# Attention followed by two expert layers: fewer filler products beside the mixed tile, expert slots of eight steps, and the first group's rows turned inside the second group's slots

## The reference

```
scores = q @ k.T / sqrt(64)                 # 2 batches, 8 heads, 576 positions, head size 64
kth    = the 32nd largest of each row
attn   = softmax(where(scores >= kth, scores, -1e9))
x      = (attn @ v), heads side by side     # 1152 rows x 512
# first expert layer: one expert of 8 for each row
logits = x @ w_gate + modality_bias[modality_id]
e      = argmax(logits);  g = softmax(logits)[e]
x      = g * (relu(x @ w1[e]) @ w2[e])      # 512 -> 1024 -> 512
# second expert layer: all 4 experts for each row
out    = sum_e p[:, e] * (relu(x @ w1b[e]) @ w2b[e])
```

## Time and profile before

| | us |
|---|---|
| median of two runs | 984.82 |
| the two runs | 984.27 and 985.36 |
| profiled execution, whole | 985.48 |
| its span | 983.7 |
| PE busy | 916.5 (93%) |
| DVE busy | 559.4 (57%) |
| ACT busy | 340.7 (35%) |
| POOL busy | 280.1 (28%) |
| mean granted TensorE clock | 0.946 |

### The profile page before, as it was taken

The page is one execution under the profiler, slowest core; times in us unless marked ns, Lnnn a source line. Parts: engine busy times, 40 slices in busy tenths (PEclk is TensorE's granted clock), DMA queues, the critical chain, the costliest instruction groups (busy, mean ns, idle before and its releaser), DMA issues.

```text
span 983.7 us, 13497 instructions
## 1 busy us (share of the span) xinstructions
PE 916.5 (93%) x4849; PEld 770.0 (78%) x4849; DVE 559.4 (57%) x1100; ACT 340.7 (35%) x726; POOL 280.1 (28%) x224
## 2 busy tenths in 40 slices
PE   4799999987799999995699979999999999999998
PEld 4688888876667767762477868998989898989897
DVE  4999999659998989834655152332314231423121
ACT  3545555433445645531645141221202120212010
POOL 7667665434657665611011030000000000000000
PEclk8579999978989999998699989999999999999999
DMA  9120000000412632533962441020202020000001
GB/s 215 57 94 22 1 23 12 12 11 21 173 34 87 214 108 97 187 114 104 330 216 101 152 179 70 1 83 4 86 1 78 9 85 0 0 0 0 32 11 53
DMA packets 49396, 75.63 MB, mean 77 GB/s; under 512 B 24624, under 2 KB 24624, under 8 KB 49328
## 3 DMA queue, kind: packets, MB, share of 16 engines
q1 hardware_dynamic: 42160, 61.09, 18.2%
q0 software_dynamic: 4160, 13.63, 4.3%
q10 hardware_dynamic: 3008, 0.05, 0.2%
HBM read 63.49 MB, written 11.27 MB: 76 GB/s over the span
## 4 chain that ended last, share of the span: by engine, by line
PE 85%; issue 5%; POOL 4%; DVE 4%; DMA 1%; ACT 1%; ACTq 0%; POOLq 0%; DVEq 0%
PE bank L1270 19%; PE bank L1271 18%; PE bank L1272 18%; PE bank L1326 9%; PE bank L1392 5%; PE bank L1367 4%; PE bank L1265 3%; PE bank L1383 3%; PE bank L1297 3%; POOL att L605 2%; PE bank L1295 2%; POOL att L608 1%; DVE w1l L1152 1%; DMA x_tok<-y_a,a_pos_i 1%; PE bank L1338 1%
## 5 line engine op out<-in xcount | busy, mean ns | idle before, releaser
L605 POOL TENSOR_SCALAR att<-sc,top 128x576 f32<-128x576 f32 x70 | 120.8, 1725 | 149.8 <-DVE top L1011 138.0
L1011 DVE MAX8 top<-work 128x8 f32<-128x576 f32 x216 | 152.4, 745 | 0.1
L1270 PE MATMUL bank<-xT,w1h 128*128 128x384 f32 x384 | 129.5, 337 | 5.3 <-DVE w1l L1152 5.3
L1271 PE MATMUL bank<-xT,w1l 128*128 128x384 f32 x384 | 129.1, 336 | 0.0
L1272 PE MATMUL bank<-xT,w1h 128*128 128x384 f32 x384 | 129.0, 336 | 0.0
L1207 DVE SCALAR_TENSOR_TENSOR hT<-bank,hT 128x384 fp32r<-128x384 f32 x96 | 53.0, 557 | 130.8 <-ACT hT L914 127.3
L914 ACT ACTIVATE hT<-bank 128x384 fp32r<-128x384 f32 x96 | 46.9, 492 | 200.9 <-PE bank L1272 200.9
L1326 PE MATMUL bank<-v_one,attT 128*128 128x65 f32 (+3 forms) x800 | 112.8, 282 | 0.6 <-ACT av L738 0.6
L1270 PE MATMUL bank<-w2h,hT 128*128 128x512 f32 x288 | 112.2, 390 | 1.2 <-DVE hT L1207 1.2
L1326 PEld LDWEIGHTS bank<-v_one,attT 128*128 128x128 f32 (+3 forms) x800 | 98.9, 190 | 17.7 <-issue 10.4
L1272 PE MATMUL bank<-w2l,hT 128*128 128x512 f32 x288 | 112.2, 390 | 0.0
(11 more groups left out here) (239 smaller groups left out, 1520.2 us busy)
## 6 DMA issues: line engine op xcount, KB each, us to landing
w_raw<-in_moe_w_dram SPq DMA_DIRECT2D x96, 512.0 KB, 5.9
q_raw<-in_q_dram SPq DMA_DIRECT2D x18, 128.0 KB, 2.7
v_one<-in_v_dram POOLq DMA_DIRECT2D x18, 128.0 KB, 5.5
out_dram<-x_tok SPq DMA_DIRECT2D x9, 256.0 KB, 2.0
k_raw<-in_k_dram SPq DMA_DIRECT2D x8, 256.0 KB, 5.2
y_dram<-zero POOLq DMA_DIRECT2D x2, 1024.0 KB, 6.6
y_dram<-b_ys POOLq DMA_DIRECT2D x7, 256.0 KB
x_dram<-x_cur SPq DMA_DIRECT2D x6, 256.0 KB, 2.8
```

Source lines behind the costliest of these rows:

```text
L605: nc.gpsimd.tensor_scalar(att[:, g % ATR, :], sc[:, g % RING, :], top8[:, g % RING, 3, 7:8], None, ALU.is_ge).then_inc(keep_made, 1)
L1011: nxt = nc.vector.max(out=top8[:, g % RING, i + 1, :], in_=work[:, j, :])
L1270: nc.tensor.matmul(dst, high_lhs, high_rhs, start=start, stop=False)
L1271: nc.tensor.matmul(dst, low_lhs, high_rhs, start=False, stop=False)
```

## The change

On PE, the number of unread products of a step depends on the tile. On DVE the counter runs with the heads themselves and advances by a seventh after each operation; the chain of group A begins at 34, asks for ranks at 36.6 and for tokens at 39.6. A's slots have eight steps and the fifth begins at step 78. `split_q` runs before the mask of head 8t and `round_q` one step earlier. SP loads the first expert's `w1` after A's fifth slot's up products. POOL gathers B's first two slots ahead of A's rows. The work on A's rows moves into B's slots: the scaling into slots 0 to 2, the turning and splitting into slots 3 to 5. `b_ys` is placed first in its region, over A's `ys`, and DVE's first copy into it waits for A's stores.

```diff
-        A_START, A_STEP, SPREAD = 46, 7, 5
+        RANKS_AT, TOKENS_AT, A_START, A_STEP, SPREAD = 37, 40, 46, 8, 5
-            return (YB, YB + 1, YB + 2, XB, HB, HB + 1)[t] if t < 2 * TB else XB
+            return (YB + 2, YB + 2, YB + 2, XB, HB, HB + 1)[t] if t < 2 * TB else XB
 # SP, end of the work beside, five slots
-                yield from clock.until(A_START + A_STEP * SPREAD + 1)
-                a_store(SPREAD - 1)
                 yield from clock.until(1000)
+                sp.wait_ge(GB.experts_made, 2)
                 with sp.If(guarded(sp, GA, SPREAD)):
...
                 with sp.Else():
+                    sp.wait_ge(a_h, 2 * SPREAD)
+                    first_up()          # load(expert_of(0), 0, w1_raw, w1, w1_split, w1_loaded)
+                    a_store(SPREAD - 1)
...
+            sp.wait_ge(slot_loaded[0], 16)
             sp.wait_ge(a_d, GA.slots)
-            load_kth(0)
+            load(expert_of(0), 0, w2_raw, w2, w2_split, w2_loaded)
 # POOL
             for g in range(HEADS - 2):
+                if g % H == 0 and g // H + 1 < T:
+                    split_q(g // H + 1)
                 mask(g)
...
-                if g % H == 1 and g // H + 1 < T:
-                    split_q(g // H + 1)
                 clock.now = g + 5
                 advance(work_beside)
-            clock.now = 1000
-            for _ in work_beside:
-                pass
             pool.wait_ge(x_kept, 16 * T)
             pool.wait_ge(GB.tokens_made, 2)
             gather_slot(0)
             gather_slot(1)
+            clock.now = 1000
+            for _ in work_beside:       # waits for a_stored, gathers A's rows
+                pass
 # ACT
-                clock.now = p if p < AV_END else STEPS - 1
+                clock.now = p
-                if p % H == 2 and p // H + 1 < T:
+                if p % H == 1 and p // H + 1 < T:
                     round_q(p // H + 1)
 # ACT, at the end of slot(s); the loops of the same before the slots are gone
+                if s < GA.tiles:
+                    act.wait_ge(gathered[s], 16)
+                    nc.scalar.activation(x_tok[:, s, :], x_tok[:, s, :], ACT.Copy, scale=GA.gate_w[:, s:s + 1]).then_inc(gated, 1)
+                elif s < 2 * GA.tiles:
+                    xT_high_part(s - GA.tiles)
 # DVE: advance() in find_thresholds is now pause()
+                def pause():
+                    advance(work_beside)
+                    clock.now += 1 / 7
+
+                clock.now = g0
...
-                yield from clock.until((GA.tiles - 1) * H + L_LAG + 1)
-                yield from route(GA, clock.until((GA.tiles - 1) * H + L_LAG + 4), clock.until((GA.tiles - 1) * H + L_LAG + 8))
+                yield from clock.until(RANKS_AT - 3)
+                yield from route(GA, clock.until(RANKS_AT - 0.4), clock.until(TOKENS_AT - 0.4))
-                clock.now = g0 + 4
 # DVE, copy_y(s) and the end of slot(s)
+                if s == 0:
+                    dve.wait_ge(a_stored, 16 * GA.slots)
+                if GA.tiles <= s < 2 * GA.tiles:
+                    xT_low(s - GA.tiles)
 # PE
-            def keep_dense(bk):
+            def dense_products(p):
+                return 4 - 2 * (p // H == SPLIT) - 2 * ((p - AV_LAG) // H == SPLIT)
+
+            def keep_dense(bk, n):
-                for i in range(4):
+                for i in range(n):
...
-                        keep_dense(MB + 2 if p < (GA.tiles - 1) * H + L_LAG + 6 else MB)
+                        keep_dense(MB + 2 if p < TOKENS_AT else MB, dense_products(p))
...
-                    a_down(s, (0, 1, 2, 3))
+                    a_down(s, (0, 1, 2))
                     yield from clock.until(at + 6)
+                    a_down(s, (3, 4, 5))
+                    yield from clock.until(at + 7)
                     if s + 1 < SPREAD:
                         a_x(s + 1)
-                    a_down(s, (4, 5, 6, 7))
+                    a_down(s, (6, 7))
 # PE, slot(s) of group B, between the turning of the hidden rows and the down products
-                if s < 2:
-                    pe.wait_ge(xT_split, GA.tiles)
-                else:
+                if GA.tiles <= s < 2 * GA.tiles:
+                    x_transposes(s - GA.tiles)
+                if s >= 2:
                     pe.wait_ge(slot_y_copied, s - 1)
 # PE, after the last step
             ranks(GB)
+            clock.now = A_START + A_STEP * SPREAD - 3
+            advance(work_beside)        # rest of the ups, both turns, downs 0 to 2 of the fifth slot
+            sum_tokens(GB)
             clock.now = 1000
             for _ in work_beside:       # downs 3 to 7
                 pass
-            sum_tokens(GB)
-            for t in range(GA.tiles):
-                x_transposes(t)
```

More of the change, by code:

```diff
@@ L191, in attention_and_experts @@
         b_mid = Region(nc, at_xT + HALF_X, at_hT)
+        b_ys = b_mid.take("b_ys", [P, 2, DM])
         b_xs_raw = b_mid.take("b_xs_raw", [P, 2, DM])
@@ L464, in a_store, with load, load_weights, expert_of @@
                 sp.dma_start(y_a[s * P:(s + 1) * P, :], ys[:, :]).then_inc(a_stored, 16)
+            def load(e, kth, raw, src, split, loaded):
+                sp.wait_ge(split, kth * DC + BASE)
+                rows = src[bass.DynSlice(e, 1)].rearrange("o (c p) f -> p (o c) f", p=P)
+                n = raw.shape[1] // DC
+                for c in range(DC):
+                    sp.dma_start(raw[:, c * n:(c + 1) * n, :], rows[:, c * n:(c + 1) * n, :]).then_inc(loaded[c], 16)
+            def load_weights(e, kth, a, b):
+                load(e, kth, w1_raw, a, w1_split, w1_loaded)
+                load(e, kth, w2_raw, b, w2_split, w2_loaded)
+            def expert_of(kth):
+                return sp.value_load(GB.kth_expert_i[0:1, bass.DynSlice(kth, 1)], min_val=0, max_val=E - 1)
+            def first_up():
+                load(expert_of(0), 0, w1_raw, w1, w1_split, w1_loaded)
             def beside():
@@ L493, in beside @@
                             sp.sem_inc(a_stored, 16)
+                    sp.wait_ge(a_d, GA.slots)
+                    first_up()
                 with sp.Else():
+                    sp.wait_ge(a_h, 2 * SPREAD)
+                    first_up()
+                    a_store(SPREAD - 1)
                     for s in range(SPREAD, GA.slots):
@@ L521, in _ @@
                 pass
[L523 to L534, removed]
             ke = sp.value_load(GB.table_i[0:1, 1, E:E + 1], min_val=1, max_val=E)
-            def load_kth(kth):
-                e = sp.value_load(GB.kth_expert_i[0:1, bass.DynSlice(kth, 1)], min_val=0, max_val=E - 1)
-                load_weights(e, kth, w1, w2)
+            sp.wait_ge(slot_loaded[0], 16)
             sp.wait_ge(a_d, GA.slots)
-            load_kth(0)
+            load(expert_of(0), 0, w2_raw, w2, w2_split, w2_loaded)
             with sp.Fori(1, E) as kth:
                 with sp.If(ke > kth):
-                    load_kth(kth)
+                    load_weights(expert_of(kth), kth, w1, w2)
             load_weights(0, ke, w1b, w2b)
@@ L790, in beside @@
                     a_copy_hT(s, 1)
-                    yield from clock.until(at + 6)
+                    yield from clock.until(at + 7)
                     if s + 1 < SPREAD:
@@ L1449, in turn_slot, with x_transposes @@
                 transposes(XB, lambda c: b_xs_raw[:, s % 2, c * P:(c + 1) * P]).then_inc(slotT_made, 1)
+            def x_transposes(t):
+                pe.wait_ge(gated, t + 1)
+                if 1 <= t < TB:
+                    pe.wait_ge(xT_split, t)
+                elif t == 2 * TB:
+                    pe.wait_ge(xT_split, TB + 1)
+                elif t > 2 * TB:
+                    pe.wait_ge(xT_split, t)
+                transposes(turned_bank(t), lambda c: x_tok[:, t, c * P:(c + 1) * P]).then_inc(xT_made, 1)
             def slot(s):
```

30 lines of the change are left out of this document (10 added, 20 removed).

## The result

| | before | changed |
|---|---|---|
| median | 984.82 | 944.57 (942.19 and 946.94) |
| ratio | 1 | 0.9591, 95% interval 0.9485 to 0.9698 |
| profiled execution, its span | 985.48, 983.7 | 946.94, 945.2 |
| mean granted clock | 0.946 | 0.96 |

Beside the experiments, on another chip, the changed kernel ran five times more: median 947.11 (945.38 to 949.78), ratio 0.9626 (0.9609 to 0.9643).

A forecast was written before the change was run, and what follows sets the result against it. PE was taken as busiest (93%), with PE and DVE idling on each other's late work around heads 32 to 45. 985.48 - 44.7 (through head 71) + 6 (clock) - 3.6 + 0.4 (end) = 943.6, forecast 943, range 931 to 960.

The forecast's parts named there:

- Part 1: Up to DVE's head 32: earlier split_q and round_q remove three PE waits for queries, worth -1.3 us.
- Part 2: DVE heads 32 to 45: later counter removes the logits and ranks waits; head 46 at 260.3, not 283.5, -23.2 us.
- Part 3: PE up to head 46: scores copied near 245, not 279.70, -34.7 us; fewer unread products keep PE from being the bound.
- Part 4: Head 46's copy to head 71's transposes: eight-step slots leave 22 rows less, 10 us; PE needs 149.8 us, ends at 394.8.
- Part 5: Clock around PE's step 40: a wait of about 5 us, then half clock for 10 to 13.6 us, costing +6 us.
- Rival 1: Steps 40 to 46: clock stays low to step 46, costing 15 us instead of 6, time 952; chance 0.16.
- Part 6: After the last head: group B's first product 36 us behind head 71's transposes, -3.6 us; transposes in B's slots +0.4 us.

## Why the prediction was right, part by part

Forecast 943, measured 944.57. The parts that carried it held, one was too small by 3.75 us, and the reason given for another failed. That the median came within 2 us is in part luck: it is that of two executions. All seven of the changed kernel lie between 942.19 and 949.78, with their median at 946.94, 4 us above the forecast, for a gain of some 38.

- **Part 1 (-1.3).** DVE started head 32 at 180.12, where 181.2 was said. PE's waits for the queries are gone. Right as a term; too small as a cause, since alone the edit is worth 20.3 us by way of PE's lead and DVE's waits.
- **Part 2 (-23.2 for DVE).** Head 46 at 261.63, forecast 260.3, before 283.5. No wait for logits or ranks in the changed kernel. Right.
- **Part 3.** "They keep PE from being the bound there" failed. With the full count PE reaches head 46 at 250.16 (248.65 and 248.47 with the turns filled as well), and with the cut at 248.22 or 254.75: PE is not the bound there with either. The cut gives PE a lead that it spends waiting, and the wait costs clock. It is worth nothing by the times (the ratio without it is 0.959), and a loss of some 4 us where the turns are filled too (0.9583 against 0.962, with intervals that just overlap).
- **Part 4 (-10 us of PE).** 149.45 us between the two marks, forecast 149.8. Right; in the second profile, with the late stretch, it was 153.4.
- **Part 5 (+6).** This step was mis-sized: the wait was 7.79 us, not 5, the stretch 30.8 us, not 10 to 13.6, and head 46's copy came 9.75 us behind the 245 of part 3. Rival 1 names what happened there (low clock to about step 44), at less than its price of 15. In the second profile the stretch was 13.6 us, as forecast, and the copy came only 3.2 us behind the 245, but a second stretch of 6.9 us near 392 cost some 3.6 us more, and head 71's transposes came at 401.62, forecast 400.8. No part of the prediction had that one.
- **Part 6 (-3.6).** 35.7 us against 36 forecast and 39.6 before. Logits 11.6 (12.2), sums 21.3 (22), splits 28.0 (29.5), but the last quarter of `w1` held the splits up by 1.35 us. Right as a sum: the early start and the late quarter nearly cancel. B's slots with the turns in them take 0.38 us more, forecast +0.4.

The profiled execution was forecast at 943.6 and took 946.94. Head 71's transposes came 3.4 us late (404.20 against 400.8), of which part 5 is +3.75 and part 4 -0.35; the rest is within 0.3.

The rule in the section "HAM oscillation — how this bites in real kernels" of the Trainium skill's page TensorE: Matmul & The Clock Gate, that waits between bursts throttle PE anew each time and more work in the burst helps, pointed the right way for the wait at step 40. In all six profiles with a wait of 5.9 to 7.8 us at step 40 or 41 the clock went to half for 13.6 us or more; with four unread products everywhere the wait was 1.48 us and the stretch 3.4, and with the turns filled too 1.17 us and none. The late stretch near 392, which had no such wait before it, does not follow from that rule.

## What to carry to other kernels

When two engines hand work to each other in fixed program order, a step counter is a promise about the other engine's lead; look up where the other engine is at that time, and expect one early question and one late answer to feed each other. Filler work has to be sized for the lead that it takes away as well as for the clock: cutting it where it seemed to be on the critical engine only moved the time into a wait here. When work is moved past a stage's end, move at the same time everything that stood behind it: the new end was worth 4 us before that move and 12 to 14 after.

## What the runs showed of the hardware

- The granted clock fell near 393 us with PE busy 6.29 of the 6.9 us before it and no idle stretch above 0.61 us, in steps of narrow products (65 columns) and transposes. That happened in two profiles; the first profile of the changed kernel had the same steps and the same 0.61 us at 394.6 and kept the full clock. With two 260-column products in each of two of these steps all three profiles kept it there. Without any unread products PE was busy without a break from 44.3 to 285.4 at half clock. Busy time is no sign of the full clock.
- After nearly the same wait (5.9 to 7.8 us at step 40 or 41) the half-clock stretch was 13.6 us in three profiles, 30.8 in two and 37.6 in one. The copy for head 46 came at 247.8 to 248.3 behind the short ones and at 254.8 to 257.5 behind the others. The kernels with this wait have a spread of 4 to 15 us between executions. Of the three with four products everywhere, and so without it, the one with bare turns has 7.5 us, the two with filled turns 2.7 and 3.4.
- A branch of SP to its Else path took about 2.6 us until the next instruction (422.85 to 425.46 in the kernel after, 456.02 to 458.66 in the kernel before). With the branch at 411.70, ahead of a wait that ended at 417.82, SP issued the load of `w1` 0.8 us behind the end of that wait, where it had been 3.9 us (422.27 to 426.20).
